# Expert weights loaded by SP from an address in a register, later raw splits, and a last product ordered by token block

## What is computed

```python
for t in range(S):                       # attention: 4 batches, 8 heads, 768 tokens, head width 48
    cur = np.einsum('bhd,bhe->bhde', u[None] * kt, vt)
    y[:, :, t] = np.einsum('bhd,bhde->bhe', rt, state + cur)
    state = w[None, :, :, None] * state + np.einsum('bhd,bhe->bhde', kt, vt)
# experts: N = 3072 tokens, width 384, E = 8, hidden 1024, each expert takes N // E = 384 tokens
logits = x @ w_gate
for idx in np.argsort(-logits.flatten()):
    tok, e = (int(idx) // E, int(idx) % E)
    if assigned[tok] >= 0 or counts[e] >= cap:
        continue
    assigned[tok] = e
    counts[e] += 1
out[mask] = np.maximum(x[mask] @ w1[e], 0.0) @ w2[e]      # mask = assigned == e
# bilinear layer: w_a, w_b are 384 x 1536, w_out is 1536 x 384
return (a * b @ w_out)                   # a = x @ w_a, b = x @ w_b
```

## Time and profile before

| | us |
|---|---|
| median of 3 runs | 864.05 (863.4 to 867.46) |
| the profiled execution | 864.73 |
| its span, first to last instruction | 863.0 |
| TensorE busy in the span | 833.5 (97%) |
| VectorE busy | 494.8 (57%) |
| GpSimd busy | 411.7 (48%) |
| ScalarE busy | 231.7 (27%) |

### The profile page before, as it was taken

One profiled execution on the slowest core, in us unless ns is written; L12 is line 12 of the kernel. 1 busy time (PEld: TensorE's weight loads), 2 busy tenths in 40 slices (PEclk: granted clock), 3 DMA queues, 4 the chain that ended last, 5 costly groups with the idle time before them and its releaser, 6 DMA issues.

```text
span 863.0 us, 17710 instructions
## 1 busy us (share of the span) xinstructions
PE 833.5 (97%) x7144; PEld 795.9 (92%) x7144; DVE 494.8 (57%) x1297; ACT 231.7 (27%) x500; POOL 411.7 (48%) x436
## 2 busy tenths in 40 slices
PE   8999997689999999999999999999999999999997
PEld 6899996479999999999999999999999999999997
DVE  7576677666665566656665666566656422641321
ACT  2343330232232223222322232223222322332222
POOL 5687871540477047704770377037703670476001
PEclk9999997799999999999999999999999999999999
DMA  9999940320122013201320131013101210121000
GB/s 160 233 236 222 223 121 30 110 65 2 50 89 65 1 51 89 65 1 49 89 65 1 50 89 64 2 50 89 56 10 49 80 55 20 62 80 61 1 1 28
DMA packets 94017, 61.72 MB, mean 72 GB/s; under 512 B 79344, under 2 KB 83952, under 8 KB 93936
## 3 DMA queue, kind: packets, MB, share of 16 engines
q0 software_dynamic: 11008, 34.61, 13.0%
q1 hardware_dynamic: 78848, 21.25, 12.8%
q10 hardware_dynamic: 4080, 4.72, 1.6%
HBM read 51.13 MB, written 9.44 MB: 70 GB/s over the span
## 4 chain that ended last, share of the span: by engine, by line
PE 91%; DVE 4%; SPq 2%; issue 1%; DMA 1%; another core or an unknown queue 0%; POOL 0%; ACT 0%; POOLq 0%; ACTq 0%; DVEq 0%
PE bank L1736 42%; PE bank L1825 17%; PE bank L1794 11%; PE bank L1508 3%; PE bank L1530 2%; SPq L455 2%; PE bank L1807 2%; PE bank L1519 2%; PE bank L1486 1%; PE bank L1772 1%; PE bank L1557 1%; PE bank L1811 1%; PE bank L1496 1%; PE bank L1568 1%; PE bank L1542 1%
## 5 line engine op out<-in xcount | busy, mean ns | idle before, releaser
L1736 PE MATMUL bank<-act,w_all 128*128 128x384 f32 x1584 | 294.8, 337 | 0.0
L1736 PEld LDWEIGHTS bank<-act,w_all 128*128 128x128 f32 x1584 | 274.8, 188 | 0.0
L1825 PE MATMUL bank<-w_all,gs 128*128 128x384 f32 x864 | 168.9, 338 | 0.1
L616 POOL DMA_INDIRECT wst<-in_moe_w,rows_i x48 | 47.7, 994 | 240.2 <-DVE rows_i L1104 217.4
L1825 PEld LDWEIGHTS bank<-w_all,gs 128*128 128x128 f32 x864 | 149.7, 188 | 0.5 <-DVE gs L1226 0.4
L633 POOL TENSOR_TENSOR w<-wst,w 128x384 fp32r<-128x384 f32 (+1 forms) x100 | 125.2, 1252 | 41.1 <-ACT w L1424 35.6
L1267 DVE TENSOR_TENSOR bank<-ga,bank 128x384 f32<-128x384 f32 x95 | 54.8, 577 | 103.3 <-PE bank L1736 97.6
L1794 PE MATMUL bank<-hs,w 128*128 128x384 f32 x576 | 112.3, 340 | 1.5 <-issue 1.5
L1794 PEld LDWEIGHTS bank<-hs,w 128*128 128x128 f32 x576 | 99.7, 188 | 1.6 <-issue 1.6
L1736 PE MATMUL bank<-act,w 128*128 128x384 f32 x504 | 99.0, 340 | 0.0
L1454 ACT ACTIVATE gs<-bank 128x384 fp32r<-128x384 f32 x95 | 46.7, 491 | 172.8 <-DVE bank L1267 172.8
(11 more groups left out here) (256 smaller groups left out, 1040.1 us busy)
## 6 DMA issues: line engine op xcount, KB each, us to landing
kt<-in_k SPq DMA_DIRECT2D x24, 192.0 KB, 4.6
rt<-in_r SPq DMA_DIRECT2D x24, 192.0 KB, 4.9
vt<-in_v SPq DMA_DIRECT2D x24, 192.0 KB, 5.1
x_rows<-xs ACTq DMA_DIRECT2D x24, 192.0 KB, 3.2
raw<-in_moe_w_a SPq DMA_DIRECT2D x6, 384.0 KB, 5.7
raw<-in_moe_w_b SPq DMA_DIRECT2D x6, 384.0 KB, 4.9
raw<-in_moe_w_out SPq DMA_DIRECT2D x6, 384.0 KB, 4.5
wst<-in_moe_w,rows_i POOLq DMA_INDIRECT x106
```

The lines of the kernel that those rows point to most:

```text
L616: pool.indirect_dma_start(parts_of(m, k)[0], None, w1_rows, bass.IndirectOffsetOnAxis(ap=rows_i[:, k:k + 1], axis=0)).then_inc(landed(m, k ...
L1736: last = pe.matmul(dst, wt(a), mv(b), start=(n == 0 and (a, b) == (0, 0)), stop=(n == len(pairs) - 1 and (a, b) == (1, 0)))
L1825: last = pe.matmul(acc[t][:, 0:D], gs2[:, c % 2, a, t * P:t * P + P], wo2[:, b, c, :], start=(c == 0 and (a, b) == (0, 0)), stop=(c == FFC ...
```

## The change

1. **SP loads the expert weights.** VectorE writes the number of the expert (`which`) instead of row numbers; SP reads it into a register (`value_load`) and issues the 14 pieces as plain transfers whose address hangs on that register, under the same conditions on `w_split`. GpSimd's indirect gathers of weights are gone, it keeps the token gathers, the splits and the stores. SP begins this after the attention's last transfer.
2. **Five pieces before the tokens.** For the first expert, ScalarE and VectorE split five pieces, not three, ahead of the tokens, and the sixth and seventh around the first hidden block.
3. **Raw splits start at block 3** and end at block 21 (before: 1 and 20).
4. **Small moves at the start.** The semaphores that start above zero are raised by GpSimd, not by SP; the gate's weights are loaded after block 3's inputs, and TensorE waits for them at its first logits. Six small constants for `rows_i` are no longer made.
5. **The last expert ends by token block.** The last product of c = 9 is put off; TensorE does the a and b products of c = 10 and 11 in a row and then for each token block the last products of c = 9, 10 and 11. The parts for c = 11 go to `LAST_GS`, a view of `hs2`, since `gs2[1]` still holds c = 9.

```diff
-        BEFORE_TOKENS, BY_POOL_0 = range(0, 3), range(10, CHUNKS)
-        UPPER_AT = {1: (6,), 2: (7, 8, 9), 3: (10, 11), 4: (12, 13)}
-        LOWER_AT = {2: (6,), 3: (7, 8, 9)}
+        BEFORE_TOKENS, BY_POOL_0 = range(0, 5), range(10, CHUNKS)
+        UPPER_AT = {1: (7,), 2: (8, 9), 3: (10, 11), 4: (12, 13)}
+        LOWER_AT = {2: (7,), 3: (8, 9)}
...
-            return 1 + p * (NT - 5) // (RAW_PIECES - 1)
+            return 3 + p * (NT - 6) // (RAW_PIECES - 1)
...
         @block.sync
         def _(sp):
-            for one in primed:
-                sp.sem_inc(one, 1)
-            sp.sem_inc(dve_step, CHAIN)
-
...
-                if n == 1:
+                if n == 3:
                     sp.dma_start(gate_w[:, :, :], w_gate.rearrange("(c p) e -> p c e", p=P)).then_inc(s_const, 16)
...
+            def load_weights(m):
+
+                sp.wait_ge(rows_ready, m + 1)
+                e = sp.value_load(which[0:1, 0:1], min_val=0, max_val=E - 1)
+                for n in range(CHUNKS):
+                    k, ahead = (n, STAGES) if m else (ORDER_0[n], FIRST_STAGES)
+                    sp.wait_ge(w_split, 1 + m * CHUNKS + max(n - ahead + 1, 0))
+                    if k < W1C:
+                        c, o = k * WIDE // F, k * WIDE % F
+                        piece = w1[bass.ds(e, 1), c * P:c * P + P, o:o + WIDE]
+                    else:
+                        piece = w2[bass.ds(e, 1), (k - W1C) * P:(k - W1C) * P + P, :]
+                    sp.dma_start(parts_of(m, k)[0], piece.rearrange("o p f -> p (o f)")).then_inc(landed(m, k), 16)
+
+            sp.wait_ge(lg_done, NT)
+            sp.wait_ge(raw_lo, RAW_PIECES)
+            for s in range(2):
+                sp.wait_ge(x_stored[s], 16 * (NT // 2))
+            for m in range(E):
+                load_weights(m)
...
+            for one in primed:
+                pool.sem_inc(one, 1)
+            pool.sem_inc(dve_step, CHAIN)
...
-            def gather_weights(m, k):
-
-                n, ahead = turn_of(m, k), STAGES if m else FIRST_STAGES
-                pool.wait_ge(w_split, 1 + m * CHUNKS + max(n - ahead + 1, 0))
-                pool.sem_inc(pool_go, 1)
-                if k < W1C:
-                    pool.indirect_dma_start(parts_of(m, k)[0], None, w1_rows,
-                                            bass.IndirectOffsetOnAxis(ap=rows_i[:, k:k + 1], axis=0)
-                                            ).then_inc(landed(m, k), 16)
...
-                pool.wait_ge(rows_ready, 1)
-                for n in range(TOKENS_AFTER):
-                    gather_weights(0, ORDER_0[n])
                 gather_tokens(0)
-                for n in range(TOKENS_AFTER, CHUNKS):
-                    gather_weights(0, ORDER_0[n])
...
-                for k in range(CHUNKS + 2):
-                    if k < CHUNKS:
-                        gather_weights(m, k)
-                    if k >= 2:
-                        split_weights(m, k - 2)
-                    if k == TOKENS_AT:
+                for k in range(CHUNKS):
+                    split_weights(m, k)
+                    if k == TOKENS_AT - 2:
                         gather_tokens(m)
...
-                dve.scalar_tensor_tensor(rows_i[:, :], row_step[:, :], top[:, 0:1], row_base[:, :],
-                                         ALU.mult, ALU.add).then_inc(rows_ready, 1)
+                dve.tensor_scalar(which[:, :], top[:, :], -1.0, float(E), ALU.mult, ALU.add).then_inc(rows_ready, 1)
...
-            lower_weights(3)
+            lower_weights(5)
             lower_hidden(0, 0)
-            lower_weights(4)
+            lower_weights(6)
             route_sums(1, 0)
-            lower_weights(5)
...
             upper_first_tokens()
-            upper_weights(0, ORDER_0[3])
+            upper_weights(0, ORDER_0[5])
             upper_hidden(0, 0)
-            upper_weights(0, ORDER_0[4])
-            upper_weights(0, ORDER_0[5])
+            upper_weights(0, ORDER_0[6])
...
+                if n == 0:
+                    pe.wait_ge(s_const, 16)
...
-            pe.wait_ge(s_const, 16)
...
-                    if c >= 1 and (more or c < FFC - 1):
+                    if not more and c == FFC - 2:
+                        pe.wait_ge(gs_lo, 1 + i * FFC + c)
+                    elif c >= 1 and (more or c < FFC - 1):
                         last_product(c - 1)
                         routing("last", c - 1)
...
-                    last_product(FFC - 2, (0, 1))
-                    last_product(FFC - 1, (0,))
-                    last_product(FFC - 2, (2,))
-                    last_product(FFC - 1, (1, 2))
+                    for t in range(CT):
+                        for c in range(FFC - 3, FFC):
+                            last_product(c, (t,))
```

More of the change, by code:

```diff
@@ L1821, in last_product @@
                 def last_product(c, ts=range(CT)):
+                    final = not more and c == FFC - 1
+                    gs = LAST_GS if final else gs2[:, c % 2, :, :]
                     for t in ts:
-                        pe.wait_ge(gs_lo, 1 + i * FFC + (c + 1) + (t if not more and c == FFC - 1 else 0))
+                        pe.wait_ge(gs_lo, 1 + i * FFC + (c + 1) + (t if final else 0))
                         for a, b in ((0, 0), (0, 1), (1, 0)):
-                            last = pe.matmul(acc[t][:, 0:D], gs2[:, c % 2, a, t * P:t * P + P], wo2[:, b, c, :],
+                            last = pe.matmul(acc[t][:, 0:D], gs[:, a, t * P:t * P + P], wo2[:, b, c, :],
                                              start=(c == 0 and (a, b) == (0, 0)),
```

28 lines of the change are left out of this document (7 added, 21 removed).

## The result

Before, 864.86 us (median of 4 runs, 863.4 to 867.46); after, **857.21 us** (4 runs, 856.34 to 858.88). The ratio is 0.9897, its 95% interval 0.9873 to 0.9921 (the quotient of these two medians is 0.9912 and lies in it). The profiled execution of after took 858.88 us (span 856.6) against 864.73 (span 863.0): 6.4 us less in the spans.

A forecast was written before the change was run, and what follows sets the result against it. TensorE was taken to bound the expert loop (busy 84.90 of 85 us), but not places the change touches. Savings of 2.1 + 0.3 + 4.4 - 0.7 + 1.0 = 7.1 us from 864.05 gave 856.9 us, range 855.2 to 863.0.

The forecast's parts named there:

- start: First few us: SP's half of the decay load issued earlier, as GpSimd raises the semaphores; -0.3 us (0 to -0.3).
- block 2: Attention block 2: TensorE's 2.07 us idle before turning block 1's output goes with later raw splits; -2.1 us (-1.7 to -2.1).
- tokens later: First expert's start: weight pieces loaded by SP beside the token gathers delay the tokens; +0.7 us (0 to +3.7).
- late signals gone, to the end of the first expert: First expert: without weight gathers TensorE's signals are heard promptly, closing gaps of 1.47 and 2.92 us; -4.4 us (0 to -4.4).
- expert loop: Loop over experts: GpSimd sheds 14 gathers per expert, but TensorE is busy 84.90 of 85 us; 0.
- end: Last expert: a and b products of c = 11 end 9 matmuls earlier, so stores start sooner; -1.0 us (-0.8 to -1.1).
- SP would issue 0.3 us earlier: Start: SP's half of the decay load, issued at 1.30 behind eight semaphore raises, goes out 0.3 us sooner.
- the first rival: First expert: late signals come from TensorE's start after idling or its own list, so 4.4 us stays: 861.3 us, chance 0.30.
- nearer to 0, because SP's six free pieces start before the tokens: First expert's tokens: reason for +0.7 us within 0 to 3.7; six pieces start early, the others wait for splits.
- whether the fifth piece is there in time: Before the tokens are lowered: fifth weight piece must land by 163.2, expected at 161.9, with 1.3 us to spare.
- the upper bound of 3.7: First expert's tokens: three weight pieces of the tokens' size taken in between at a 1.25 us pitch cost 3.7 us.
- The second rival: First expert: shared DMA engines or slow SP issue delay token gathers or the fifth piece; 865.5 us, chance 0.10 (cost above 3.7).

The follow-up runs named there:

- the run with late splits: The changed kernel with GpSimd's last six splits of each expert from the second on started later, and SP raising the starting semaphores again: 857.99 us.
- The loads alone: The kernel before with only the expert weights loaded by SP at a register address instead of gathered by GpSimd: 857.94 us against 867.46, ratio 0.9888.
- after's second profile: The changed kernel rerun unaltered in a second group of runs: 857.34 us, ratio 0.9965 to the kernel before.
- dummy gathers: The changed kernel plus eight unread gathers of 64 bytes a row by GpSimd behind the first expert's token gathers: 862.41 us.

## Why the prediction was right, and where only its sum was

The forecast was 856.9 us and the time is 857.21; the spans differ by 6.4 where the sum said 7.1. Terms by the marks in both traces (first `ktok`, end of block 2, end of attention, last `ids_done`, last token turned, L1654 against L1640, the experts' `yt_done`, third store):

| place | predicted | measured |
| --- | --- | --- |
| start | -0.3 | +0.20 |
| block 2 | -2.1 | -2.26, later +0.16 |
| last `ids_done` heard sooner | none | -0.93 |
| tokens later | +0.7 (0 to 3.7) | +2.43 |
| slower clock of the first up parts | none | +1.78 |
| late signals gone, to the end of the first expert | -4.4 | -4.95 |
| expert loop | 0 | -1.77 |
| end | -1.0 | -1.02 |
| sum | -7.1 | -6.4 |

**Start.** The step "SP would issue 0.3 us earlier" held: its half of the decay goes out at 0.98. The gain didn't follow in after:

```profile
3.26 0.21 DVE L689 COPY decay_rev<-decay 128x4 f32<-128x4 f32 x1 [1.71 <-DMA decay<-in_w]
```

VectorE is released 0.11 us later than in the earlier trace rows. With SP's issue back at 1.30 (the run with late splits) the release is at 3.17, but that first operation takes 0.29 us instead of 0.17, and the chain behind it is as late. The loads alone settle whose the +0.20 is: there SP raises the semaphores as in before and issues at 1.31, and the release (3.17), the first operation (0.29) and the first `ktok` (10.36 for 10.16) are those of the run with late splits. So the small moves at the start were worth 0.01 us, and the 0.20 came with the loads' part of the change; by which of its edits isn't shown. The step that failed took the issue for the landing.

**Block 2.** Right in place, mechanism and size. The +0.16 behind it is no more than chance: in after's second profile the rest of the attention gave 0.65 us instead. What the prediction missed: in two of three profiles of kernels with before's raw splits and gathers the gap costs 3.3 us more, by its own length and the clock.

**The late signals.** "By coincidence in time, not by a proof" was the right reading, and is now shown: dummy gathers bring the lateness back, and without the weight gathers it is gone, worth 4.6 us in the loads alone. What TensorE does may have a part in it all the same, as the first rival says, since only signals of dense products came 2 us late or more. Read the same way, the routing's last `ids_done` was late as well (VectorE waits 1.3 to 1.4 us for it in all traces with the weight gathers and 0.5 in all without): gone, it gave 0.9 us that the prediction hadn't looked for. The first rival (0.30), by which the change would leave both gaps, falls. The Trainium skill's page "DMA: Bandwidth & Descriptors" (Issuing engines are not separate DMA queues), by which a change of issuer saves only issue time, doesn't cover this: the loads alone gave 9.5 us by the medians and 7.4 by the profiled spans.

**Tokens.** The step that was mis-sized is the +0.7: "nearer to 0, because SP's six free pieces start before the tokens". They did; but the splits ahead of the tokens also set the next pieces free in the midst of the gathers, three at 158.47 and, by the fourth and fifth split, two more at 160.81. With the three alone the tokens cost 1.1 us. The prediction checked whether the fifth piece is there in time (it was) and not what its split triggers. It cost 2.4 us, and 1.8 more by the clock, together 4.2, beyond the upper bound of 3.7. The second rival's cause was real at half its price.

**The loop.** "Worth 0, with 84.90 of 85 us at work" was read from one stretch, 280 to 365 us. A loss of 0.35 us an expert is 0.4% of it, and the rows of matmuls, whose ends are modelled, show only 0.4 us of idle time for it over the whole loop. Of the 1.77 some 1.2 are the costly hits, which three of the four traces with gathers in the loop have and none of the ten with the loads: a gain that nobody foresaw, and one that an execution of before can have without the change. TensorE's share can't bound such a term below half a us per expert.

**The end.** Right to the tenth: the third store starts 6.36 us early, the sixth expert's end 5.34.

That the total fits is partly luck: 4.2 us of unforeseen cost (start, attention, tokens, clock) against 3.4 of unforeseen gain.

## What to carry to other kernels

When a step moves forward, list what its semaphore sets free, and ask which transfer that lands on: holding back the first expert's seventh and later pieces by one wait gave 3.5 us, about half of what the whole change gave. Keep GpSimd's gathers from running back to back where TensorE hands over small results, and look at hearers' times, not only at the idle engine. And price a wait of TensorE by the matmuls behind it as well: twice here (block 2, first up parts) the clock fell after waits of 1.2 to 2.7 us, and the work behind took nearly twice as long. It doesn't fall after every such wait, so look at the granted clock of several executions.

## What was new about the hardware

- TensorE's signals behind dense products were heard up to 5.3 us late while GpSimd worked through back-to-back gathers, and 5.1 us with gathers of 64 bytes a row; without them they were heard within 0.04 us (after's two hidden blocks). Signals of the small transposes just before, with the same gathers running, were prompt.
- With waits of 1.16 and 1.37 us between the token blocks the clock fell to 1.2 GHz for 6.8 us; with fillers between them it didn't. With waits of 2.06 and 1.50 us in another run it stayed up, so the length of a wait doesn't settle it. In block 2 it stayed up behind gaps of 1.38 and 2.07 us and fell behind 2.71 us, twice; there too for 6.8 us.
- An operation of VectorE on two SBUF inputs, begun 0.04 us behind a GpSimd subtraction, took 1.11 us for 0.28; begun 0.04 us ahead, 0.28. In before's loop such hits came back in four experts one after the other.
